# Half tiles in pairs and later first-layer weights in the opening stage of a retention and two-MLP kernel on one core

## What is computed

```python
scores = scale * np.matmul(q, k.transpose(0, 1, 3, 2))
ret = scores * Dmat[None, :, :, :]                      # decay gamma ** (i - j), zero above the diagonal
x = np.matmul(ret, v)  ->  (1152, 512)
p = domain_probs / (domain_probs.sum(-1, keepdims=True) + 1e-09)
for e in range(4):                                      # w1[e]: 512 x 1024, w2[e]: 1024 x 512
    h = np.maximum(x @ w1[e], 0.0)
    out += p[:, e:e + 1] * (h @ w2[e])
h = x @ w_in                                            # w_in: 512 x 2048, w_out: 2048 x 512
g = h * np.tanh(log1p(exp(h)))
out = g @ w_out
```

## Time and profile before

| | |
|---|---|
| median of 3 runs | 626.48 us (626.34 to 626.99) |
| profiled execution | 627.09 us, span 625.2 us |
| PE busy | 618.1 us (99% of the span), 3773 matmuls |
| PE weight load, DVE, ACT, POOL busy | 553.7, 271.6, 237.0, 285.0 us |
| granted clock of PE in the 40 slices | 9 tenths or more in each |
| DMA | 50.43 MB, of them 144 weight loads of 256 KB and 18 chunks of 512 KB |

### The profile page before, as it was taken

How to read it: one execution, slowest core, us unless ns; L and a number is a source line. 1 busy time by engine, 2 the same in 40 slices (tenths; PEclk the granted TensorE clock), 3 DMA queues, 4 the chain that set the end, 5 groups by cost and what they waited for, 6 DMA issues and landing times.

```text
span 625.2 us, 9507 instructions
## 1 busy us (share of the span) xinstructions
PE 618.1 (99%) x3773; PEld 553.7 (89%) x3773; DVE 271.6 (43%) x388; ACT 237.0 (38%) x459; POOL 285.0 (46%) x239
## 2 busy tenths in 40 slices
PE   8999999999999999999999999999999999999997
PEld 5788899999999999999999899988989999989996
DVE  5646854433154433154433154434545432324334
ACT  3446423432223432123442223435455454334431
POOL 4657645553435542535543635532435553443300
PEclk9999999999999999999999999999999999999999
DMA  8955312332102321212312212321211233201002
GB/s 271 318 185 174 106 48 68 101 89 63 51 35 68 102 79 57 68 35 67 102 67 69 69 35 67 88 81 35 68 34 35 68 117 85 68 0 52 1 0 102
DMA packets 25147, 50.43 MB, mean 81 GB/s; under 512 B 2896, under 2 KB 3216, under 8 KB 25104
## 3 DMA queue, kind: packets, MB, share of 16 engines
q1 hardware_dynamic: 24816, 49.66, 25.4%
q10 hardware_dynamic: 288, 0.17, 0.1%
HBM read 47.45 MB, written 2.36 MB: 80 GB/s over the span
## 4 chain that ended last, share of the span: by engine, by line
PE 97%; DMA 1%; DVE 1%; issue 0%; ACT 0%; SPq 0%; DVEq 0%; ACTq 0%
PE bank L494 31%; PE bank L496 30%; PE bank L495 30%; PE bank L448 2%; PE bank L488 2%; DMA qkv<-in_chunks 1%; PE bank L619 1%; PE bank L452 1%; PE bank L626 0%; DVE acc_sb L895 0%; DVE acc_sb L899 0%; ACT qkv L696 0%; DVE qkv L822 0%; DVE h_lo L856 0%; SPq L418 0%
## 5 line engine op out<-in xcount | busy, mean ns | idle before, releaser
L395 POOL TENSOR_TENSOR w_lo<-w_raw,w_hi 128x512 fp32r<-128x512 f32 x96 | 132.2, 1389 | 150.7 <-ACT w_hi L368 148.9
L494 PE MATMUL bank<-w_hi,h_hi 128*128 128x512 f32 x432 | 168.8, 391 | 0.0
L496 PE MATMUL bank<-w_hi,h_lo 128*128 128x512 f32 x432 | 168.4, 390 | 0.0
L495 PE MATMUL bank<-w_lo,h_hi 128*128 128x512 f32 x432 | 168.3, 390 | 0.0
L882 DVE TENSOR_TENSOR h_act<-part,bank 128x384 f32<-128x384 f32 x96 | 52.9, 552 | 169.7 <-PE bank L496 168.9
L390 POOL TENSOR_TENSOR ws<-ws_f,ws 128x1024 fp32r<-128x1024 f32 x24 | 57.6, 2400 | 145.1 <-ACT ws L364 145.1
L496 PEld LDWEIGHTS bank<-w_hi,h_lo 128*128 128x128 f32 x432 | 81.1, 188 | 16.9
L495 PEld LDWEIGHTS bank<-w_lo,h_hi 128*128 128x128 f32 x432 | 81.1, 188 | 12.3
L494 PEld LDWEIGHTS bank<-w_hi,h_hi 128*128 128x128 f32 x432 | 81.0, 188 | 12.2
L732 ACT ACTIVATE part<-bank 128x384 f32<-128x384 f32 x72 | 35.4, 491 | 139.3 <-PE bank L496 139.3
L849 DVE SCALAR_TENSOR_TENSOR h_lo<-h_act,h_hi 128x384 fp32r<-128x384 f32 x64 | 74.3, 1170 | 20.6 <-ACT h_hi L722 20.0
(11 more groups left out here) (87 smaller groups left out, 911.4 us busy)
## 6 DMA issues: line engine op xcount, KB each, us to landing
w_raw<-in_weights SPq DMA_DIRECT2D x144, 256.0 KB, 2.8
qkv<-in_chunks SPq DMA_DIRECT2D x18, 512.0 KB, 4.6
out<-acc_sb SPq DMA_DIRECT2D x6, 256.0 KB, 2.0
out<-acc_sb SPq DMA_DIRECT2D x1, 768.0 KB, 3.6
consts<-in_consts ACTq DMA_DIRECT2D x1, 146.0 KB, 3.6
ident<-in_consts SPq DMA_DIRECT2D x1, 64.0 KB, 4.0
consts<-in_consts SPq DMA_DIRECT2D x1, 34.0 KB, 3.9
p_nat<-in_probs ACTq DMA_DIRECT2D x1, 18.0 KB, 3.6
```

The lines of the kernel that those rows point to most:

```text
L395: pool.tensor_tensor(w_lo[layer][:, x], w_raw[:, r % RAW], w_hi[layer][:, x].bitcast(F32), ALU.subtract).then_inc(s_wl, 1)
L494: pe.matmul(out, w[0], x[0], start=first, stop=False, **more)
L495: pe.matmul(out, w[0], x[1], start=False, stop=False, **more)
L496: return pe.matmul(out, w[1], x[0], start=False, stop=last, **more)
```

## The change

The half tiles stand behind the scores alone, except for the first one, in turn 7. Turns 8, 10, 12 and 14 have two in a row, the other turns up to 18 have one. The weights of the eight tiles are loaded with chunks 7, 9 and 11 to 16 (before: 6 to 13), one of the second layer with chunk 17, and split in turns 5, 7, 9, 10, 11, 12, 13 and 13 (before: 5 to 12). The second layer's first three jobs are in turns 14, 15 and 15 (before: 12, 13, 14).

```diff
-AFTER_SCORES = {8: (0, 1), 9: (1, 1), 10: (2, 1), 11: (3, 1), 12: (4, 1), 13: (5, 0), 14: (5, 1),
-                15: (6, 0), 16: (6, 1), 17: (7, 0), 18: (7, 1)}
-AFTER_OUTPUT = {7: (0, 0), 8: (1, 0), 9: (2, 0), 10: (3, 0), 11: (4, 0)}
+FIRST_HALF_IN = 7
+HALVES_IN = {8: (1, 3), 9: (3, 4), 10: (4, 6), 11: (6, 7), 12: (7, 9), 13: (9, 10), 14: (10, 12),
+             15: (12, 13), 16: (13, 14), 17: (14, 15), 18: (15, 16)}
...
+WEIGHTS_WITH = {7: 0, 9: 1, 11: 2, 12: 3, 13: 4, 14: 5, 15: 6, 16: 7, 17: 8}
+W1_IN = (5, 7, 9, 10, 11, 12, 13, 13)
...
-        add(IN_TURN, 5 + u, "w1", 0, u)
+        add(IN_TURN, W1_IN[u], "w1", 0, u)
     for u in range(3):
-        add(IN_TURN, 12 + u, "w2", 0, u)
+        add(IN_TURN, 14 + (u + 1) // 2, "w2", 0, u)
...
-            for c in range(2, 6):
+            for c in range(2, CHUNKS):
                 if c > 2:
                     chunk_there(c - 3)
                 load_chunk(c)
...
+                if c in WEIGHTS_WITH:
+                    load_weights(WEIGHTS_WITH[c])
...
-                if c in AFTER_SCORES:
-                    plain_half(*AFTER_SCORES[c])
+                for n in range(*HALVES_IN.get(c, (0, 0))):
+                    plain_half(n // 2, n % 2)
                 keep_warm(WARM_IN.get(c, 0))
                 if c > 0:
                     output(c - 1)
-                if c in AFTER_OUTPUT:
-                    plain_half(*AFTER_OUTPUT[c])
+                if c == FIRST_HALF_IN:
+                    plain_half(0, 0)
```

More of the change, by code:

```diff
@@ L60 @@
 HS = HEADS // 2
-AFTER_SCORES = {8: (0, 1), 9: (1, 1), 10: (2, 1), 11: (3, 1), 12: (4, 1), 13: (5, 0), 14: (5, 1),
-                15: (6, 0), 16: (6, 1), 17: (7, 0), 18: (7, 1)}
-AFTER_OUTPUT = {7: (0, 0), 8: (1, 0), 9: (2, 0), 10: (3, 0), 11: (4, 0)}
-HIDDEN_IN = {t: c for c, (t, half) in AFTER_SCORES.items() if half}
+FIRST_HALF_IN = 7
+HALVES_IN = {8: (1, 3), 9: (3, 4), 10: (4, 6), 11: (6, 7), 12: (7, 9), 13: (9, 10), 14: (10, 12),
+             15: (12, 13), 16: (13, 14), 17: (14, 15), 18: (15, 16)}
+HIDDEN_IN = {n // 2: c for c, span in HALVES_IN.items() for n in range(*span) if n % 2}
 ROWS_IN = {0: 4, 1: 5, 6: 6, 7: 7, 8: 8}
+WEIGHTS_WITH = {7: 0, 9: 1, 11: 2, 12: 3, 13: 4, 14: 5, 15: 6, 16: 7, 17: 8}
+W1_IN = (5, 7, 9, 10, 11, 12, 13, 13)
 WARM_IN = {0: 3, 6: 8}
@@ L424, in _ @@
                 load_chunk(c)
[L425 to L433, removed]
+                if c in WEIGHTS_WITH:
+                    load_weights(WEIGHTS_WITH[c])
             sp.dma_start(ident[:, :], consts_in[:, CONSTS:]).then_inc(s_id, 16)
-            for r in range(UNITS + CHUNKS - 6 - UNITS, len(LOADS)):
+            for r in range(len(WEIGHTS_WITH), len(LOADS)):
                 load_weights(r)
```

## The result

| | before | changed kernel |
|---|---|---|
| median of 6 runs each | 626.84 us (626.34 to 630.25) | 635.27 us (633.95 to 636.95) |
| ratio to before, 95% interval | | 1.0127 (1.0099 to 1.0155) |
| profiled execution, and its span | 627.09, 625.2 us | 635.99, 634.2 us |

The account below looks back on a forecast made before the run. PE, busy for 99% of the span, bounds the kernel. Pairs -0.8, stop in turn 6 -0.7, weights one turn ahead +4.8 and late sums +2.7 gave +6.0 us: 626.48 + 6.0 = 632.5 us, range 629.3 to 635.0.

Parts of the forecast that it names:

- One sign of being wrong that the forecast gave: The forecast called itself wrong if, among other signs, the granted clock was below 1.00 behind a stall.
- Pairs of halves: Turns 8, 10, 12 and 14: a half right behind another saves 0.2 us of one entry and exit; -0.8 us.
- The stop in turn 6: PE's 1.07 us stop among matmuls of zeros shrinks with fewer weight loads ahead; -0.7 us, bounds 0 to -1.4.
- smaller stops: Some 0.3 us of PE stops in turns 3 and 4, added to the turn 6 stop's bound of gain.
- Waits of turns 10, 11 and 12: PE waits for low parts of weights made one turn ahead: 2.0, 2.0 and 0.8 us, sum +4.8 us.
- The chain of 3.63 us against 1.70 us of cover: Turn 10: low part ends 3.63 us after the output's start, PE wants it after 1.70; 2.0 us wait.
- the forecast's 40.4 us for the whole pass: First half to second layer: 36.41 + 4.8 - 0.8 = 40.4 us.
- The late sums: Two low parts in turn 15 make POOL's sums of weights 3.0 us later, so P6 waits +2.7 us.
- The rival by which this stall would not come: Ahead of P6: better turns of POOL and DVE at the port shrink the delay; 629.8 us, chance 0.2.
- The sum of lowest terms: Whole forecast's low end: -0.8 - 1.4 + 3.9 + 2.2 = +3.9 us, or 630.4 us.
- POOL's and ACT's jobs of turn 6 fall away there, which nobody waits for: Turn 6: the removal of these weight jobs was given no cost or gain of its own.
- The clock, chance 0.07: Rival: PE's clock falls in the stalls, 1.5 us per fall, three falls 4.5 us: 637 us, chance 0.07.

Follow-up runs that it names:

- e1: Changed kernel with the weight splitting of tiles 2, 3 and 4 one turn earlier: 628.82 us, 1.0049 of before.
- e2: Kernel before with the new places of the half tiles alone, weight jobs and loads as before: 626.30 us, 0.9986 of before.
- e6: Kernel before with the new places of the halves and weight load u with chunk u + 7 instead of u + 6: 625.68 us, 0.9976 of before.
- e9: Changed kernel repaired: halves kept, weight splits and some loads earlier, v of chunk 9 behind the low part of turn 6's output: 625.04 us, 0.9963 of before.
- e10: The e6 kernel (new halves, old jobs, loads one chunk later) once more on another chip: 626.43 us, 0.9982 of before.
- e3: Changed kernel, with POOL in turn 7 waiting for the low part of turn 6's output before scaling v of chunk 9: 636.14 us, 1.0155 of before.
- e4: Changed kernel with seven matmuls of zeros ahead of the halves of turn 10: 635.25 us, 1.0147 of before.
- e5: Changed kernel with tile 6's weights split in turn 12 and the second layer's first three in 13, 14, 14: 633.78 us, 1.0096 of before.
- e8: Changed kernel with matmuls of zeros in each long wait (turns 10, 11, 12 and ahead of P6): 633.02 us, 1.0092 of before.
- e7: Kernel before with weight load u with chunk u + 7 instead of u + 6, nothing else: 626.74 us, 1.0004 of before.

## Why the forecast held, and where not

The direction and the two main places of the loss were right. The value was 2.4 us too low (8.4 for 6.0): the median of the runs, 635.27, lies just above the range's 635.0, the ratio times the 626.48 of before, 634.4, just inside. That it is inside owes something to luck: the range took in half a fall of the clock, and the runs had one or two. One sign of being wrong that the forecast gave came true, the granted clock below 1.00 behind a stall (0.56).

- **Pairs of halves, -0.8 forecast: -1.0.** e1, e2, e6, e9 and e10 all show 35.4 us for 36.4. By that an entry and an exit cost 0.25 us, not the 0.2 that I took from one half.
- **The stop in turn 6, -0.7 forecast, within 0 to -1.4: -1.4 in the profile**, the far end of its bounds. It is a draw: six profiles (changed kernel, e1, e3, e4, e5, e8) share loads and program there, and less their waits in turn 7 the stretch is 1.0 to 1.5 us shorter than before's in five and 0.15 longer in e4, where the stop was there in full; 1.0 shorter on average. Of the 0.3 us of smaller stops that were put to its bounds, only 0.15 are "until issue"; the rest are waits for DVE and ACT.
- **Waits of turns 10, 11 and 12, 2.0 + 2.0 + 0.8 forecast: 1.90, 2.00, 0.69.** The chain of 3.63 us against 1.70 us of cover was the right view: in the changed kernel it is 3.61 us in turn 10 and 3.55 in turn 11. e1 takes the waits away with nothing but the turn of the jobs. That e8 has exactly the forecast's 40.4 us for the whole pass is luck: pairs and waits were 0.4 us less than forecast, and the 0.4 of restarts were not in it.
- **The late sums, 2.7 forecast: 2.33 of waiting, 2.5 of time.** Sums 2.66 us later instead of 3.0, 0.2 us of slack instead of 0.3; e5 shows the proportion. The path was right up to its last step: P6 was to be released by ACT's copy of P1, and was by DVE's last low part of the sums of x, 0.09 us behind it. The rival by which this stall would not come falls. (The sum of lowest terms has 2.2 us for this one, the text beside it a bound of 0.)
- **"POOL's and ACT's jobs of turn 6 fall away there, which nobody waits for": the step that failed in turn 7.** Nobody waited for the job, but POOL waited behind it, and its next step of v had been kept out of DVE's way by it. Priced at nothing, it cost 0.6 us; e3 shows it by DVE's 0.41 us for 1.14.
- **The clock, chance 0.07: it fell in every run.** This is the main miss. The row that spoke against it was a stop of 1.07 us, and I let that speak for waits of 1.9 to 2.7 us, which it can't. The price was right (1.5 us a fall, measured 1.56), three falls were too many at once for this kernel (two of e3's four runs had them): the case to name was one or two, at 633 + 1.6 to 3.2 us by the profiled run, and it deserved most of the chance.

Summed up: 6.0 forecast; pairs -0.2 and stop -0.7 against it, turn 7 +0.6, turns 10 to 12 and P6 -0.4 together, some +0.4 of restarts: 5.7, or 6.1 with the stop's average over six profiles; e8, which has no falls, measures 6.1. So the 6.0 of the forecast for a kernel without falls was right in part because errors of 0.2 to 0.6 us cancelled. The falls bring the other 2.2. The 1.6 us by which turn 0 begins late in the profiled run are no part of it, and without the table of segments they would have passed for a loss.

## What to carry to other kernels

When a use moves ahead, measure the chain from what triggers its producer to its last step, and the work that covers it; every us that is missing is a wait, and it repeats in each turn that hangs on the one before. Look at what stands behind a job that is taken out of an in-order engine: it moves up, and may run beside the one step that somebody waits for. Where the bounding engine's clock falls in its waits, as PE's did here, a wait of about 2 us is dearer than its length: price the fall with it, or keep the engine busy through the wait.

## What the hardware did that was not expected

- **The clock can fall at one idle time of 1.9 us.** In the profiled executions falls came with idle times of 1.89 to 1.91 (turn 10), 1.97 to 1.98 (turn 11) and 2.33 to 2.37 us (P6), in stretches otherwise at full work. They began between 0.4 us before and 1.0 us after the end of the idle time, lasted 3.41 us each and cost 1.4 to 1.6. With idle times of 0.6 to 1.34 us there was none. It did not fall at each long one, but at eight of eleven: the changed kernel's profile has it in turn 10 and not in turn 11 (2.00 us) or at P6, e3's in all three places. What decides is open, and so is what made it fall in the few runs of before, e6, e7 and e10. The Trainium skill, "TensorE: Matmul & The Clock Gate", section "Why this matters for your kernels", warns of idle gaps between bursts of matmuls, but of longer ones than any here. The runs agree that gaps bring the clock down, and differ in the length: a single gap of 1.9 us in full work was enough.
- **Filling a wait pays.** Zeros through all the waits cost nothing that shows and gave 2.2 us back (e8); through one wait alone they gave nothing, since the next wait brought the fall (e4).
- **DVE's subtraction waited until POOL's running instruction was over.** With two SBUF inputs and 0.41 to 0.43 us of its own it took 1.14 and 1.26 us when it started behind a 64x512 step of POOL, and one of 0.38 us took 1.93 to 1.95 beside the 2.4 us low part of the sums. Each ended 0.15 to 0.3 us behind POOL's instruction. One that started 0.08 us ahead of POOL's step took its usual 0.42 us (DVE at 16.69 and POOL at 16.77 us in the kernel before). In the changed kernel:

```profile
70.87 1.95 DVE L842 TENSOR_TENSOR xb_lo<-xf,xb_hi 128x128 fp32r<-128x128 f32 x1 [3.53 <-ACT xb_hi L701]
```

```profile
70.26 2.41 POOL L396 TENSOR_TENSOR ws<-ws_f,ws 128x1024 fp32r<-128x1024 f32 x1 [1.24 <-ACT ws L370]
```

- **The clock's rise at the start varies** from 4.4 to 10.7 us in executions that are alike up to there, and turn 0 starts up to 1.7 us later where it is late.
